# Chunked attention ahead of two MoE layers: scores and weighted sums computed per head on 64 rows of TensorE instead of per pair of heads on 128

## The reference

```python
B, H, S, D = q.shape          # 4, 8, 768, 64
chunk, left_ctx, right_ctx = (32, 16, 8)
for c in range(S // chunk):
    ...
    k_full = np.concatenate([mem_k, k_ctx], axis=2)
    v_full = np.concatenate([mem_v, v_ctx], axis=2)
    scores = scale * np.matmul(q_c, k_full.transpose(0, 1, 3, 2))
    scores = scores - np.max(scores, axis=-1, keepdims=True)
    a = np.exp(scores)
    a = a / (np.sum(a, axis=-1, keepdims=True) + 1e-09)
    out[:, :, c_start:c_end] = np.matmul(a, v_full)
```

## Time and profile before

| | |
|---|---|
| time, median of 3 runs (lowest to highest) | 752.46 us (749.99 to 753.69) |
| the profiled execution's own time | 749.99 us |
| its span, first to last instruction | 748.2 us |
| TensorE busy | 716.0 us, 96% of the span |
| VectorE busy | 323.5 us, 43% |
| ScalarE busy | 229.6 us, 31% |
| GpSimd busy | 125.0 us, 17% |
| HBM read and written | 79.77 MB and 16.79 MB |

### The profile page before, as it was taken

The page is one execution under the profiler, slowest core; times in us unless marked ns, Lnnn a source line. Parts: engine busy times, 40 slices in busy tenths (PEclk is TensorE's granted clock), DMA queues, the critical chain, the costliest instruction groups (busy, mean ns, idle before and its releaser), DMA issues.

```text
span 748.2 us, 13078 instructions
## 1 busy us (share of the span) xinstructions
PE 716.0 (96%) x5059; PEld 587.2 (78%) x5059; DVE 323.5 (43%) x569; ACT 229.6 (31%) x363; POOL 125.0 (17%) x153
## 2 busy tenths in 40 slices
PE   5999965999999999979999999999999999999998
PEld 4777642999999999958888888888888888888886
DVE  4777767566656666535332222222221222222212
ACT  4554523455555555533221111111111111111011
POOL 7211113224555344410000000000000000000000
PEclk9999985999999999999999999999999999999999
DMA  8999955656576665454002000300030021001001
GB/s 288 413 315 311 349 185 181 183 200 212 186 242 209 204 195 178 151 198 204 0 1 76 37 1 1 112 1 1 0 112 0 0 62 50 0 0 57 0 1 56
DMA packets 31114, 93.01 MB, mean 124 GB/s; under 512 B 5036, under 2 KB 5164, under 8 KB 30320
## 3 DMA queue, kind: packets, MB, share of 16 engines
q1 hardware_dynamic: 27792, 87.65, 33.9%
q0 software_dynamic: 3296, 5.00, 2.0%
HBM read 79.77 MB, written 16.79 MB: 129 GB/s over the span
## 4 chain that ended last, share of the span: by engine, by line
PE 93%; DVE 3%; DMA 2%; issue 1%; ACT 1%; POOL 0%; SPq 0%; DVEq 0%; POOLq 0%
PE ps_m L1062 14%; PE ps_m L1064 13%; PE ps_m L1063 13%; PE ps_f L1064 4%; PE ps_f L1063 4%; PE ps_f L1062 4%; PE ps_h L1062 4%; PE ps_h L1064 4%; PE ps_h L1063 4%; PE ps_y L1062 4%; PE ps_y L1063 4%; PE ps_y L1064 4%; PE ps_o L1004 3%; PE ps_s L957 3%; PE ps_pT L969 2%; PE ps_xT L991 2%
## 5 line engine op out<-in xcount | busy, mean ns | idle before, releaser
L1062 PE MATMUL ps_m<-f_xhi,fin_lo 128*128 128x512 f32 x432 | 170.7, 395 | 1.4 <-DVE f_xlo L902 1.4
L1064 PE MATMUL ps_m<-f_xhi,fin_hi 128*128 128x512 f32 x432 | 170.6, 395 | 0.0
L1063 PE MATMUL ps_m<-f_xlo,fin_hi 128*128 128x512 f32 x432 | 170.5, 395 | 0.0
L852 DVE TENSOR_TENSOR w_lo<-raw,w_hi 128x1024 fp32r<-128x1024 f32 x67 | 82.0, 1225 | 62.4 <-ACT w_hi L624 62.4
L912 DVE TENSOR_TENSOR f_b<-ps_m,f_a 128x512 f32<-128x512 f32 x36 | 24.9, 692 | 178.6 <-PE ps_m L1064 178.5
L1062 PEld LDWEIGHTS ps_m<-f_xhi,fin_lo 128*128 128x128 f32 x432 | 81.1, 188 | 21.1 <-DVE f_xlo L902 1.7
L1064 PEld LDWEIGHTS ps_m<-f_xhi,fin_hi 128*128 128x128 f32 x432 | 81.1, 188 | 19.6
L1063 PEld LDWEIGHTS ps_m<-f_xlo,fin_hi 128*128 128x128 f32 x432 | 81.1, 188 | 19.6
L624 ACT ACTIVATE w_hi<-raw 128x1024 fp32r<-128x1024 f32 x67 | 71.0, 1059 | 53.7 <-PE ps_y L1064 50.5
L660 ACT ACTIVATE f_hhi<-f_h 128x512 fp32r<-128x512 f32 x36 | 22.8, 632 | 206.7 <-DVE f_h L915 206.7
L1062 PE MATMUL ps_h<-x_hi,w_lo 128*128 128x256 f32 x256 | 73.0, 285 | 2.2 <-DVE x_lo L859 2.2
(11 more groups left out here) (149 smaller groups left out, 950.9 us busy)
## 6 DMA issues: line engine op xcount, KB each, us to landing
raw<-wpack SPq DMA_DIRECT2D x67, 512.0 KB, 4.2
v_sb<-vW SPq DMA_DIRECT2D x32, 390.0 KB, 5.4
k_sb<-kT SPq DMA_DIRECT2D x32, 250.0 KB, 4.9
q_sb<-qT SPq DMA_DIRECT2D x16, 384.0 KB, 5.9
x_dram<-x_buf SPq DMA_DIRECT2D x4, 1536.0 KB, 11.3
fin_raw<-wfin SPq DMA_DIRECT2D x6, 1024.0 KB, 12.0
f_in<-x_dram SPq DMA_DIRECT2D x5, 1024.0 KB, 5.4
out<-f_out SPq DMA_DIRECT2D x5, 1024.0 KB, 4.2
```

The lines of the kernel that those rows point to most:

```text
L852: dve.tensor_tensor(w_lo[c % RING][:, :], raw[:, c % RAW, :], w_hi[c % RING][:, :].bitcast(F32), ALU.subtract).then_inc(s_wlo, 1)
L1062: pe.matmul(out_, a_lo, b_hi, start=first, stop=False)
L1063: pe.matmul(out_, a_hi, b_lo, start=False, stop=False)
L1064: return pe.matmul(out_, a_hi, b_hi, start=False, stop=end)
```

## The change

Each head now has a matmul of its own on 64 rows: q and k of head 0 lie on partitions 0 to 63, those of head 1 on 64 to 127, and likewise for the probabilities and v. A matmul has 64 rows, 32 columns of weights and 64 moving columns (65 for the sums), and there are twice as many. Head 0 writes one PSUM bank and head 1 another; `ps_s` and `ps_o` are now one tensor of two banks each, in place of two tensors used in turn. So the scores of a group wait for the subtraction of the group just before (`s_diff`, n in place of n-1), and the sums wait for the normalization of the group just before (`s_xn`, likewise). Before each of these two blocks PE increments a semaphore (`order`), an instruction that now carries the waits. There are no zero blocks, so their writes and the waits for them are gone. k and v come with one load of 128 partitions each in place of two of 64, with the same bytes.

```diff
+            q_sb = [sb(f"q_sb{i}", [P, S]) for i in range(SETS)]
+            k_sb = [sb(f"k_sb{i}", [P, KCOLS]) for i in range(SETS)]
+            v_sb = [sb(f"v_sb{i}", [P, NCH, DV]) for i in range(SETS)]
-            ps_s = [ps(f"ps_s{i}", [P, TPG, 2, WIN]) for i in range(2)]
+            ps_s = ps("ps_s", [P, 2, BANK])
-            ps_o = [ps(f"ps_o{i}", [P, TPG, 2, DV]) for i in range(2)]
+            ps_o = ps("ps_o", [P, 2, BANK])
...
+        def scores(rows):
+            return ps_s[rows, :, 0:TPG * WIN].rearrange("p h (t w) -> p h t w", t=TPG)
+        def sums(rows):
+            return ps_o[rows, :, 0:TPG * DV].rearrange("p h (t d) -> p h t d", t=TPG)
+        def head(h):
+            return slice(D * h, D * h + D)
...
-                if n < SETS:
-                    sp.wait_ge(s_zk[i], 1)
-                else:
+                if n >= SETS:
                     sp.wait_ge(s_score, (n - SETS + 1) * GROUPS)
-                for h in range(2):
-                    sp.dma_start(k_sb[i][h:P:2, h, :], kT[b, j, h]).then_inc(s_qk[i], 16)
+                sp.dma_start(k_sb[i][:, :], kT[b, j]).then_inc(s_qk[i], 16)
...
-            dve.memset(zero[:, :], 0.0).then_inc(s_zt, 1)
-            dve.memset(k_sb[0][:, :, :], 0.0).then_inc(s_zk[0], 1)
-            dve.memset(v_sb[1][:, 0, :, :], 0.0).then_inc(s_zv[1], 1)
...
-                    dve.tensor_tensor(prob[g % 2][:, :, :, :].rearrange("p t w h -> p t h w"), scores,
...
+                    dve.tensor_tensor(prob[g % 2][:, :, :, :].rearrange("p t h w -> p h t w"), scores(slice(0, P)),
+                                      maxima.unsqueeze(3).to_broadcast([P, 2, TPG, WIN]), ALU.subtract).then_inc(s_diff, 1)
...
+            def order():
+                pe.sem_inc(s_carry, 1)
...
-                    if not isinstance(b, int) or n >= 2:
-                        pe.wait_ge(s_diff, n - 1)
+                    if not isinstance(b, int) or n >= 1:
+                        pe.wait_ge(s_diff, n)
+                    order()
                     for t in range(TPG):
                         for r in range(QT):
                             c = (u * TPG + t) * QT + r
-                            last = pe.matmul(ps_s[g % 2][CHUNK * r:CHUNK * (r + 1), t, :, :],
-                                             q_sb[j][:, c * CHUNK:(c + 1) * CHUNK],
-                                             k_sb[j][:, :, c * BLOCK:c * BLOCK + WIN], start=True, stop=True)
+                            for h in range(2):
+                                last = pe.matmul(scores(slice(CHUNK * r, CHUNK * (r + 1)))[:, h, t, :],
+                                                 q_sb[j][head(h), c * CHUNK:(c + 1) * CHUNK],
+                                                 k_sb[j][head(h), c * BLOCK:c * BLOCK + WIN], start=True, stop=True)
...
-                    if not isinstance(b, int) or n >= 2:
-                        pe.wait_ge(s_xn, n - 1)
+                    if not isinstance(b, int) or n >= 1:
+                        pe.wait_ge(s_xn, n)
+                    order()
...
+                            for h in range(2):
+                                last = pe.matmul(sums(slice(CHUNK * r, CHUNK * (r + 1)))[:, h, t, :],
+                                                 probT[head(h), t, CHUNK * r:CHUNK * (r + 1)],
+                                                 v_sb[j][head(h), c, :], start=True, stop=True)
```

More of the change, by code:

```diff
@@ L32 @@
 GW = TPG * P
+BANK = 512
 DV = D + 1
@@ L107, in build @@
             x_buf = sb("x_buf", [P, NTT, DM])
-        with ExitStack() as early:
-            sb, _ = tensors(early)
-            far = [(sb(f"q_sb{i}", [P, S]), sb(f"k_sb{i}", [P, 2, KCOLS]), sb(f"v_sb{i}", [P, 2, NCH, DV]))
-                   for i in (2, 3)]
         sb, _ = tensors(ctx)
@@ L135, in build @@
             sb, ps = tensors(att)
-            near = [(sb(f"q_sb{i}", [P, S]), sb(f"k_sb{i}", [P, 2, KCOLS]), sb(f"v_sb{i}", [P, 2, NCH, DV]))
-                    for i in range(2)]
-            q_sb, k_sb, v_sb = zip(*(near + far))
-            prob = [sb(f"prob{i}", [P, TPG, WIN, 2]) for i in range(2)]
+            q_sb = [sb(f"q_sb{i}", [P, S]) for i in range(SETS)]
+            k_sb = [sb(f"k_sb{i}", [P, KCOLS]) for i in range(SETS)]
+            v_sb = [sb(f"v_sb{i}", [P, NCH, DV]) for i in range(SETS)]
+            prob = [sb(f"prob{i}", [P, TPG, 2, WIN]) for i in range(2)]
             xn = [sb(f"xn{i}", [P, TPG, P]) for i in range(2)]
@@ L235, in build @@
         s_const = sem("s_const")
-        s_zt = sem("s_zt")
-        s_zk = [sem(f"s_zk{i}") for i in range(SETS)]
-        s_zv = [sem(f"s_zv{i}") for i in range(SETS)]
         s_w9 = sem("s_w9")
@@ L245, in build @@
         s_pass = sem("s_pass")
+        s_carry = sem("s_carry")
         s_score = sem("s_score")
@@ L457, in _ @@
         def _(pool):
-            for h in range(2):
-                pool.memset(v_sb[0][:, h, :, :], 0.0).then_inc(s_zv[0], 1)
             pool.memset(ident[:, :], 0.0).then_inc(s_pc, 1)
@@ L483, in routing_constants @@
                               allow_small_or_imprecise_dtypes=True).then_inc(s_rc, 1)
-            def clear(i):
-                pool.memset(k_sb[i][:, :, :], 0.0).then_inc(s_zk[i], 1)
-                for h in range(2):
-                    pool.memset(v_sb[i][:, h, :, :], 0.0).then_inc(s_zv[i], 1)
-            clear(2)
             def keep_x(b, s):
                 if isinstance(b, int) and b == 0:
-                    if s == 1:
-                        clear(3)
-                    if s == 5:
+                    if s == 3:
                         routing_constants()
@@ L968, in attend @@
                     for t in range(TPG):
-                        last = pe.transpose(ps_pT[:, t * P:(t + 1) * P], prob[g % 2][:, t, :, :].rearrange("p w h -> p (w h)"),
+                        last = pe.transpose(ps_pT[:, t * P:(t + 1) * P], prob[g % 2][:, t, :, :].rearrange("p h w -> p (h w)"),
                                             ident[:, :])
@@ L1003, in attend @@
                             c = (u * TPG + t) * QT + r
-                            last = pe.matmul(ps_o[g % 2][CHUNK * r:CHUNK * (r + 1), t, :, :],
-                                             probT[:, t, CHUNK * r:CHUNK * (r + 1)],
-                                             v_sb[j][:, :, c, :], start=True, stop=True)
+                            for h in range(2):
+                                last = pe.matmul(sums(slice(CHUNK * r, CHUNK * (r + 1)))[:, h, t, :],
+                                                 probT[head(h), t, CHUNK * r:CHUNK * (r + 1)],
+                                                 v_sb[j][head(h), c, :], start=True, stop=True)
                     last.then_inc(s_o, 1)
@@ L1184 @@
     arrays = {
-        "qT": c(q.reshape(B, PAIRS, 2, S, D).transpose(0, 1, 4, 2, 3).reshape(B, PAIRS, P, S)),
-        "kT": c(keys.transpose(0, 1, 3, 2).reshape(B, PAIRS, 2, D, KCOLS)),
-        "vW": value_windows(window_blocks(v, mem_v)).reshape(B, PAIRS, 2, WIN, NCH * DV),
+        "qT": c(q.reshape(B, PAIRS, 2, S, D).transpose(0, 1, 2, 4, 3).reshape(B, PAIRS, P, S)),
+        "kT": c(keys.transpose(0, 1, 3, 2).reshape(B, PAIRS, P, KCOLS)),
+        "vW": value_windows(window_blocks(v, mem_v)).reshape(B, PAIRS, P, NCH * DV),
         "w9": c(np.concatenate([moe_w_gate, moe_w_skip[:, None], np.zeros((DM, W9 - E - 1), moe_w_gate.dtype)], 1)
```

40 lines of the change are left out of this document (15 added, 25 removed).

## The result

The changed kernel takes 814.09 us (median of 4 runs, 813.52 to 815.14), the kernel before 753.08 (4 runs, 749.99 to 755.36): a ratio of 1.0815, 95% interval 1.0773 to 1.0856. It is 61 us slower, and the forecast was 741 with a range of 736 to 749. The profiled execution took 813.52 us, with a span of 811.5 against 748.2.

What follows compares the result with a forecast made beforehand. TensorE was taken to bound attention, VectorE next. Gains of 8.5 us in steps, 3.0 at the start and 0.3 in the drain, 11.8 together, gave 738.2 from the profiled 750.0, or 740.7 against the median: 741, range 736 to 749.

Steps and rivals of the forecast that it cites:

- instructions don't come fast enough: Rival for TensorE in attention: pieces of program come too late, steps of 4 us in first-time steps, 760 us; chance 0.08.
- the 16 steps that run for the first time: Attention steps in which that supply rival lost 15 us, against 3 gained at the start and 4 in later steps.
- The clock stays 1.00: Sign expected in the profile after: TensorE's granted clock in attention stays at 1.00, the level of 2.4 GHz.
- The halved matmuls: TensorE's scores and sums with 64 columns: each block loses 0.32 us, TensorE's own step falls from 2.77 to 2.08.
- Six waves: A block of scores or sums: 48 passes in waves of eight, six waves of 0.053 us if row halves run side by side.
- 0.05 on a gap: TensorE's weight-load gap between blocks of different shape: 0.2 us falls to 0.15 after a 64-column wave.
- the 7.1 of the sum: Gain in us of attention's 23 ordinary steps, 0.31 each, from 2.76 to 2.45.
- The loop of waits: Single-buffer waits between TensorE and VectorE in attention: two steps take 2.53 + 2.33 = 4.86 us, 2.43 a step, taken as 2.45.
- The start: Attention's start without zero writes: keys land at 5.0 us, group 2's subtraction ends 3.0 us earlier, bounds 2.0 and 3.5.
- The loads stayed hidden: Attention's loads: a pair takes 4.1 us, two steps would take 4.9, leaving a margin of 0.8 us a pair.
- the rivals that end slower: Late instructions (760 us, 0.08), every pass issued in turn (787, 0.03) and the clock staying low (769, 0.03); summed as 0.11.
- the 769 of the low clock: Rival for TensorE in attention: clock at 1.2 GHz, step near 3.4 us, +19, 769 us; chance 0.03.

Runs made afterwards that it cites:

- Experiments one: Kernel before, with each matmul of scores and sums issued as two of half the width, by head, on 128 rows: 812.22 us, ratio 1.0777.
- two: Kernel before, with only the scores' matmuls split in two by head, 174 TensorE instructions a step: 763.68 us, ratio 1.0133.
- five: Kernel before with only the scores split and TensorE's loop written out, so each instruction runs once: 777.75 us, ratio 1.0313.
- six: Kernel before with TensorE's loop written out, 126 instructions a step, nothing else changed: 755.27 us, ratio 1.0013.
- Experiment four: Changed kernel with scores and sums computed in one pass from the upper 16 bits, 128 instructions a step: 765.43 us, ratio 1.0164.
- experiment nine: Scores per head on row halves as in the changed kernel, sums in the old form with zero blocks, heads on partition halves: 780.3 us, ratio 1.0367.
- experiment eight: Changed kernel with only the sums in one pass from the upper 16 bits, 176 instructions a step: 760.52 us, ratio 1.0093.
- experiment three: Kernel before with one buffer each for scores and sums, the changed kernel's waits and two semaphore increments: 756.08 us, ratio 1.0032.
- experiment ten: Kernel before, its matmuls and loop, but each head on 64 neighbouring partitions so loads needn't wait for zeros: 772.96 us, ratio 1.0265.
- experiment seven: Changed kernel with q, k and v loaded for batch 0 only: 824.84 us, total not comparable; attention ends at 145.57 against 161.17.

## Why the prediction was wrong, step by step

- **The step that failed is the supply of instructions.** It was a rival, "instructions don't come fast enough", with 0.08 and 760 us. Its condition was read rightly (a piece each 2.65 to 3.0 us would be wanted), and its evidence wrongly: 1.2% of 16 queues over 38 us is 1.0 us of *transfer* a piece, and I took the transfer for the time that a piece takes. What the earlier trace rows has besides, 7 pieces in 38 us or 5.4 us each, is the pace at which that kernel asked: it uses up a piece in 5.8 us. That it ran without stops said nothing of reserve, and no row of before shows where the limit is. Experiments one, two, five and six show it: no loss at 5.8 us wanted for a piece, a loss from 4.2 on, and about 5.3 us each on average is what comes. The transfer is 1.0 us of that; what the rest is stays open.
- **Its price was mis-sized too.** I let only the 16 steps that run for the first time lose. A loop of 1786 instructions is not kept, and all 29 steps lose: 64 us, not 15. Experiment two against the changed kernel bounds the size: kept at 1393, not at 1786. The Trainium skill, Runtime: NRT & Kernel Launch, "Instruction fetch mechanics", has blocks of 256 instructions, which the stops here show, and calls the crossing of one mostly hidden, which 40.9 us of stops here contradict.
- **"The clock stays 1.00" failed as a consequence.** It is 0.77 from 60 to 97 us: it falls to 1.2 GHz again and again in this stage, where the kernel before, with TensorE busy 36.97 of 37, held 2.4. In 20 to 140 us about 23.5 steps ran. At 2.6 each they would take 61, the stops 41; the other 18 us of 120 are what the low clock and the restarts cost, an estimate. Experiment four shows the low clock without stops, 3.3 a step, with cheaper passes.
- **The halved matmuls were half right.** The row halves run side by side, eight passes in 0.056 us. "Six waves" holds for four; the last 16 passes of a block start one after another. The term was 0.64 us gained on the two blocks and 0.05 on a gap; measured, the two together give back 0.15, and TensorE's step is 2.60 and not 2.08. In experiment nine the scores' part of it was lost again on the way from the sums to the scores. With this alone, and no stops, the gain would have been 0.16 a step, some 4 us over the 23 ordinary steps in place of the 7.1 of the sum: an estimate.
- **The loop of waits had the right form** where it could be seen: 0.15 for the scores after the subtraction (experiment eight). Its terms for the two blocks were 0.34 us too small in 4.86. The steps of 2.38 to 2.46 there, with cheaper sums, are near 2.43 because VectorE bounds them, and don't bear the loop out. The single buffers cost 0.01 us a step (experiment three).
- **The start was right in size:** 2.3 us at group 2, where 3.0 was taken, with bounds of 2.0 and 3.5. Keys landed at 5.7 and not 5.0. An early start bought with loads of 64 neighbouring partitions is another matter: in experiment ten the first subtraction ended 0.9 earlier than before, and group 2's 0.9 later.
- **The loads stayed hidden**, as argued; without them the stage is some 16 us shorter, for the most part by shorter stops: 1.3 us a step in place of 1.7 (experiment seven).
- **Two slips in the sums** change nothing above: the rivals that end slower have 0.08 + 0.03 + 0.03 = 0.14 together, not 0.11; and the 769 of the low clock is 19 on the profiled execution's 750.0, where the other rivals start from 752.5.

## What to carry to other kernels

Count an engine's instructions per microsecond before splitting its operations: here TensorE lived with 126 in 2.8 us, and with 222, wanted in 2.6 or less, it stood still a third of the time, whatever the queue's busy share said. Read from the profile how often pieces of program come, not how long their transfer takes, and ask whether a loop's second round fetches at all; a loop that has grown past what is kept pays in every round. And when a change cuts streaming columns without cutting instructions, don't take the block's time to shrink with them: measure a block on the timeline of both kernels, on the same kind of row, and look at the granted clock.

## What the runs showed of the hardware that was not expected

- TensorE's program comes in pieces of 256 instructions, about 5.3 us apart on average under loads (21 in 111 us, experiment five) and 4.9 without (from steps of 4.24 us, experiment seven), and the engine stops dead at the piece's end, in the midst of a block.
- A loop of 1009 or 1393 TensorE instructions is fetched once; one of 1786 in every round.
- Of 48 passes on eight small tiles 32 start mostly 7 ns apart, and most of the other 16 at 16 to 17 ns.
- TensorE can be "busy" 90% of a stage at 1.2 GHz (experiment four, 45.16 us of 50, with transposes of 440 ns in place of 291).
- Loads into 64 neighbouring partitions moved 221 to 249 GB/s with full queues, on one queue or two; from 14 to 19 us 238, where loads into every second partition moved 412.
